# Experts' tokens sorted while attention runs, experts' weights held stationary under 416 streamed rows, and last-layer outputs scattered by token

## The reference, cut to what matters

```python
for t in range(S):                      # B=4, H=8, S=768, D=48; r, k, v: [B, H, S, D]
    cur = einsum('bhd,bhe->bhde', u * kt, vt)
    y[:, :, t] = einsum('bhd,bhde->bhe', rt, state + cur)
    state = w[:, :, None] * state + einsum('bhd,bhe->bhde', kt, vt)
x = y.transpose(0, 2, 1, 3).reshape(3072, 384)        # 3072 tokens
logits = x @ w_gate                                   # 8 experts
e_idx = argmax(logits, axis=1)                        # one expert for each token
gate_w = softmax(logits)[e_idx];  eom = sigmoid(x @ w_output_gate)[e_idx]
for e in range(8):                                    # w1: 384 x 1024, w2: 1024 x 384
    ye = maximum(x[e_idx == e] @ w1[e], 0) @ w2[e]
    x2[e_idx == e] = gate_w * eom * ye
g = x2 @ w_gate2                                      # d_ff = 1536
out = (g * sigmoid(g) * (x2 @ w_val)) @ w_out         # float32
```

## Time and profile before

| | us |
|---|---|
| time, median of 3 runs | 996.05 |
| lowest and highest run | 994.66, 996.93 |
| span of the profiled execution, first to last instruction | 962.4 |

### The profile page before, as it was taken

How to read it: one execution, slowest core, us unless ns; L and a number is a source line. 1 busy time by engine, 2 the same in 40 slices (tenths; PEclk the granted TensorE clock), 3 DMA queues, 4 the chain that set the end, 5 groups by cost and what they waited for, 6 DMA issues and landing times.

```text
span 962.4 us, 19802 instructions
## 1 busy us (share of the span) xinstructions
PE 905.8 (94%) x6919; PEld 856.9 (89%) x6920; DVE 416.5 (43%) x697; ACT 255.9 (27%) x511; POOL 341.3 (35%) x276
## 2 busy tenths in 40 slices
PE   6899998898998999999979999999999999999998
PEld 6777787697897888988878999999999999999998
DVE  7767766536655547264244222222232223222221
ACT  1333332122222222222233222222222222222222
POOL 6799996577444326065346010010100001000000
PEclk9999999999999999999999999999999999999999
DMA  8885565353324132224221010000100001000000
GB/s 198 224 223 129 129 163 186 85 167 113 133 85 155 39 133 82 82 62 150 93 80 29 22 42 9 25 25 0 49 0 25 25 18 31 0 25 0 25 1 25
DMA packets 115583, 74.20 MB, mean 77 GB/s; under 512 B 79248, under 2 KB 109840, under 8 KB 115552
## 3 DMA queue, kind: packets, MB, share of 16 engines
q1 hardware_dynamic: 101312, 48.01, 18.2%
q10 hardware_dynamic: 10720, 14.95, 4.3%
q0 software_dynamic: 3520, 10.82, 4.0%
HBM read 57.44 MB, written 16.32 MB: 77 GB/s over the span
## 4 chain that ended last, share of the span: by engine, by line
PE 67%; POOL 12%; issue 7%; DVE 6%; DMA 3%; POOLq 2%; DVEq 1%; SPq 1%; ACT 1%; ACTq 0%
PE bank L1187 20%; PE bank L1189 20%; PE bank L1188 20%; POOL w_lo L501 3%; POOL w_lo L552 3%; DMA xs<-x_rows,token_of 2%; POOL k_pad L486 2%; POOL r_pad L488 2%; POOL ruk L491 2%; PE bank L1239 1%; PE bank L1083 1%; POOL xs L531 1%; POOLq L549 1%; SPq L401 1%; DVE w_hi L832 1%
## 5 line engine op out<-in xcount | busy, mean ns | idle before, releaser
L1187 PE MATMUL bank<-bT_hi,f_hi 128*128 (+1 forms) x576 | 194.7, 338 | 0.0
L1188 PE MATMUL bank<-bT_lo,f_hi 128*128 (+1 forms) x576 | 192.8, 335 | 0.0
L1189 PE MATMUL bank<-bT_hi,f_lo 128*128 (+1 forms) x576 | 192.6, 334 | 0.0
L890 DVE TENSOR_TENSOR act<-silu,bank 128x384 f32<-128x384 f32 x96 | 53.2, 554 | 252.1 <-PE bank L1189 252.1
L552 POOL TENSOR_TENSOR w_lo<-raw,w_hi x72 | 99.0, 1408 | 111.1 <-DVE w_hi L832 107.0
L571 POOL DMA_INDIRECT xg<-y_slots,slot_of x24 | 25.0, 1040 | 277.4 <-DVE xg_s L874 256.2
L1188 PEld LDWEIGHTS bank<-bT_lo,f_hi 128*128 128x128 f32 x576 | 108.5, 188 | 0.0
L1187 PEld LDWEIGHTS bank<-bT_hi,f_hi 128*128 128x128 f32 x576 | 108.4, 188 | 0.0
L1189 PEld LDWEIGHTS bank<-bT_hi,f_lo 128*128 128x128 f32 x576 | 108.4, 188 | 0.0
L1187 PE MATMUL bank<-f_hi,act_hi 128*128 128x384 f32 x288 | 96.8, 336 | 2.5 <-DVE act_lo L893 2.5
L1189 PE MATMUL bank<-f_hi,act_lo 128*128 128x384 f32 x288 | 96.7, 336 | 0.0
(11 more groups left out here) (169 smaller groups left out, 1464.6 us busy)
## 6 DMA issues: line engine op xcount, KB each, us to landing
raw<-in_moe_w_dram SPq DMA_DIRECT2D x16, 1536.0 KB, 6.7
y_slots<-y_out ACTq DMA_DIRECT2D x28, 192.0 KB, 1.9
k_in<-in_k_dram SPq DMA_DIRECT2D x24, 192.0 KB, 2.7
r_in<-in_r_dram SPq DMA_DIRECT2D x24, 192.0 KB, 3.5
v_in<-in_v_dram SPq DMA_DIRECT2D x24, 192.0 KB, 3.7
x_rows<-x_out ACTq DMA_DIRECT2D x24, 192.0 KB, 1.9
out_dram<-o_out ACTq DMA_DIRECT2D x7, 576.0 KB, 3.0
f_raw<-in_moe_w_gate_dram SPq DMA_DIRECT2D x12, 192.0 KB, 2.6
```

The costliest lines, as they stand in the source:

```text
L890: dve.tensor_tensor(act[:, par, :], silu[:, par, :], bank[2 * par + 1][:, 0:BN], ALU.mult).then_inc(act_made, 1)
L1187: pe.matmul(ps, a_hi, b_hi_, start=first, stop=False)
L1188: pe.matmul(ps, a_hi, b_lo_, start=False, stop=False)
L1189: return pe.matmul(ps, a_lo, b_hi_, start=False, stop=last)
```

## The change

**During attention.** `x_out` holds three chunks, with room for 16 logits behind each row of 384. After each chunk of four steps, VectorE picks the experts of its 512 tokens (`choose`), TensorE counts ranks with three small matmuls (`ranks`), VectorE turns them into row numbers (`place`), and GpSimd scatters the rows with their logits into `x_sorted` in DRAM, a region of 3584 rows for each expert (`store_rows`, one indirect DMA a step, 16 of them between attention steps and 8 behind them). Only one expert's weights are split in attention, in eight chunks of 768 columns, in steps 4 to 11. The attention loops are unrolled.

**Between.** Counts of the tokens give tables of windows of 416 rows. SP writes 416 rows of zeros behind each expert's last row, the first expert's ahead of the first load of rows, the other seven behind it. The one-hot inversion and the gathers are gone.

**Experts.** `window_rounds` loops over windows. A window's rows are loaded as [104, 4] rows by a plain DMA, scaled by their gates at once (`scale_of`, `scale_rows`), transposed by 12 small transposes and split. `up(j, f)` and `down(j, f)` hold 128x128 blocks of the weights stationary and stream the 416 rows, 9 matmuls each; the hidden layer comes out transposed as `down` needs it. All weights of an expert are loaded and split in eight chunks, in the window before. With seed 0 the reference's arithmetic gives the experts 380, 348, 359, 410, 409, 389, 374 and 403 tokens (28 tiles of 128, as the kernel before uses), so each has one window. During the first window GpSimd also issues 24 indirect DMAs that write each sorted row's token number to `token_at` (`place_token`).

**Last layer.** The outputs stay on chip (`y_all`, transposed), so nothing is stored, gathered or transposed. Six blocks of 512 sorted rows; `gate_and_val` streams 512 columns, into the same two PSUM banks each time; `to_out` does 12 matmuls of 384 columns. GpSimd scatters each output tile to `out` by the token numbers (`store_out`).

The diff, cut to its core:

```diff
-    BT = 3
-    BN = BT * P
+    WP, WT = 104, 4
+    W = WP * WT
+    REGION = 3584
+    ROW = DM + 2 * E
+    BN = 512
+    BT = BN // P
...
+            fill(0, first_filled)
+            sp.wait_ge(first_filled, 16)
+            for n in range(XBUF):
+                for b in range(B):
+                    sp.wait_ge(x_stored[n][b], 16 * CH // XBUF)
+            load_rows(0)
+            for e in range(1, E):
+                fill(e, rest_filled)
+            sp.wait_ge(tables_made, 1)
+            end = last_window(sp)
+            sp.wait_ge(rest_filled, 16 * (E - 1))
+            with sp.Fori(1, end + 1, 1) as j:
+                row = sp.value_load(window_row[0:1, bass.ds(j, 1)], min_val=0, max_val=E * REGION - W)
+                sp.wait_ge(xs_made, WT * j)
+                load_rows(row)
+                e = sp.value_load(window_expert[0:1, bass.ds(j, 1)], min_val=0, max_val=E - 1)
+                for f in range(FC1):
+                    sp.wait_ge(w_split, FC1 * j + (f - RAW + 1))
+                    load_chunk(e, f)
...
-                if not at_end(c, 0):
-                    lo_piece(i - B)
+                if SPLIT_AT <= i < SPLIT_AT + FC1:
+                    lo_chunk(0, i - SPLIT_AT)
...
+            for i in range(STEPS):
+                attention_step(i)
+                for n in STORE_AFTER.get(i, ()):
+                    store_rows(n)
...
+            for j, first, last in window_rounds(pool, end):
+                for f in range(FC1):
+                    if f < SPLIT_LAG and not first:
+                        lo_chunk(j, FC1 - SPLIT_LAG + f)
+                    if f >= SPLIT_LAG and not last:
+                        lo_chunk(j + 1, f - SPLIT_LAG)
+                    if first:
+                        for t in range(f * NT // FC1, (f + 1) * NT // FC1):
+                            place_token(t)
+                if first:
+                    pool.wait_ge(tokens_placed, 16 * NT)
...
+            set_routing_up()
+            for i in range(STEPS):
+                attention_step(i)
+                if i >= B and i % B == 1:
+                    choose(i // B - 1)
+                if i >= B and i % B == 2:
+                    place(i // B - 1)
+            choose(CH - 1)
+            place(CH - 1)
...
+            for j, first, last in window_rounds(dve, end):
+                for f in range(FC1):
+                    hidden_lo(j, f)
+                    if f == 1 and not first:
+                        y_copy(j - 1)
+                    if not last:
+                        if f == 0:
+                            scale_of(j + 1)
+                        if f in (1, 2):
+                            scale_rows(j + 1, range((f - 1) * WT // 2, f * WT // 2))
+                        if f in COPY_AT:
+                            x_lo(j + 1, COPY_AT.index(f))
...
+            def up(j, f):
+                pe.wait_ge(w_split, FC1 * j + (f + 1))
+                wait(pe, h_lo_made, FC1 * j + (f - 1))
                 for c in range(KC):
+                    mm = three_passes(bank[f % 2][:, 0:W], w_hi[:, f, at], w_lo[:, f, at],
+                                      window_of(xT_hi, j, c), window_of(xT_lo, j, c), c == 0, c == KC - 1)
...
-                wait(pe, act_made, i - 1)
+                wait(pe, act_made, i)
```

More of the change, by code:

```diff
@@ L867, in _ @@
[L867 to L877 removed]
+            dve.tensor_tensor(place_i[:], place_f[:], slot_f[:], ALU.add).then_inc(places_made, 1)
@@ new lines, in _ @@
+            for c in range(KC):
+                rows_turn(0, c)
+            stay_warm(WARM_FIRST, bank[0])
+            pe.wait_ge(tables_made, 1)
+            end = last_window(pe)
+            for j, first, last in window_rounds(pe, end):
+                for f in range(FC1):
+                    up(j, f)
+                    if f in TURN_AT and not last:
+                        rows_turn(j + 1, TURN_AT.index(f))
+                    if f >= 2:
+                        down(j, f - 2).then_inc(down_mm, 1)
+                    elif not first:
+                        down(j - 1, FC1 - 2 + f).then_inc(down_mm, 1)
```

1192 lines of the change are left out of this document (523 added, 669 removed).

## The result

The changed kernel took 1016.46 us (median of four runs, 1015.08 to 1019.49) beside 995.36 for the kernel before (993.85 to 996.93): ratio 1.0229, 95% interval 1.0200 to 1.0258. It is slower; 921 was forecast, with a range of 901 to 945.

A forecast was written before the change was run, and what follows sets the result against it. TensorE was taken as the main bound, with GpSimd holding attention. The terms 10 + 0 - 57 - 15.9 - 15 + 2.5 = -75.4 took the 962.4 span to 887.0; plus 33.65 outside it, 921 us, range 901 to 945.

The forecast's parts named there:

- Step 1: Attention: GpSimd loses 20 pieces and gains eight wider subtractions and 16 scatters between steps; +10 us.
- Step 2: Routing, from the last `x_out` to the first expert matmul: 24.8 us before and after, change 0, bounds 20 and 29.
- Step 3: Experts: 297.0 to 240 us, -57, from 223.8 of TensorE work and 16.5 of holes.
- (a): First expert window: the second load of rows stands behind seven zero fills, leaving TensorE about 8.5 us idle.
- (c): First expert window: GpSimd's 24 token scatters delay its splits, so the third window's rows come late; 4 us.
- (b): Experts: TensorE's clock drops after the wait before the first window and after (a); twice about 2 us.
- rival B: Late rows hold every expert window, 3.7 us in each of six: 22 us, so 943; chance 0.17.
- Step 4: Hand-over between expert layers: store, gather, scale and transposes go; 18.2 to 2.3 us, -15.9.
- Step 5: Last layer: 72 steps of 6.18 us, fewer matmuls and transposes; 461.2 to 446 us, -15.
- Rival D: Last layer: one pair of PSUM banks makes TensorE wait in each of 72 steps, slower than before; chance 0.04.
- Step 6: The end: four copies, then four scatters 1.30 apart, the last landing 3.3 after its start; 3.8 to 6.3 us, +2.5.
- C: Attention takes its upper bound, VectorE's loop up to about 6 us in steps with `choose`: +14, so 935; chance 0.16.

The follow-up runs named there:

- e1: The changed kernel with GpSimd's weight subtraction in attention one step behind ScalarE's cast; 972.6 us, ratio 1.006 to the kernel before.
- e6: e5_four with each of the 16 scatters in attention one step later; 933.8 us, ratio 0.943 to the kernel before.
- e8: e6 with two buffers for ruk in turn instead of one; 905.1 us, ratio 0.940 to the kernel before.
- e11: e10_spread with two buffers for ruk in turn; 906.4 us, ratio 0.939 to the kernel before.
- e7: e6 with room for four chunks in x_out, so 8 scatters stand between attention steps and 16 behind; 908.0 us, ratio 0.942 to the kernel before.
- e12_best: e6 plus two ruk buffers, room for four chunks in x_out and spread token writes; 898.8 us, ratio 0.930 to the kernel before.
- e2: The changed kernel with the next window's rows issued behind the fifth of eight chunk loads, not the eighth; 976.1 us, ratio 1.008 to the kernel before.
- before_again: The kernel before run once more in the second series, nothing edited; 994.9 us.
- e5_four: The changed kernel with subtraction a step later, next window's rows earlier, token numbers written in the last layer, six zero fills behind window 1's rows; 939.0 us.
- e6_again: e6 run once more in a later series, nothing edited; 913.3 us, ratio 0.944 to the kernel before.
- e10_spread: e6 with the 24 token writes three behind each of the eight late weight slices; 912.4 us, ratio 0.947 to the kernel before.

## Why the prediction was wrong, step by step

**Step 1, attention, +10: the step that failed most, +67.9 measured.** It failed in "It gains eight subtractions of 768 columns, 1.5 times as wide, 2.2 each: +17.6". The subtractions took 1.80 us each, less than the 2.2, and the scatters were near (1.28 to 1.30). What is missing is the wait: I counted the subtraction as busy time of GpSimd and never asked what it waits for, nor who waits for what stands behind it. The diff shows both: `lo_piece(i - B)` became `lo_chunk(0, i - SPLIT_AT)`, the same index as ScalarE's cast, and the cast stood behind `logits_copy`. That is 37 us on the last `x_out` (e1). Of the other 21 over the forecast, some 8 went when the scatters moved a step on (e6; the wait for row numbers that I had as a bound came to 5.0 in e1), 6 to 7 with the second ruk buffer (e8, e11), and scatters taken out of the steps gave 9 (e7); the last `x_out` of one kernel moves by up to 3 us between runs. The floor of 4.4 us a step from the earlier trace rows, 5.7 with a scatter, did not hold as a floor of the step: the twelve steps behind the circle took 6.95 on average, since GpSimd's work is one part of a loop with VectorE and TensorE. e12_best's 164.0 is under the 167.4 forecast, with eight scatters instead of 16 inside.

**Step 2, routing, 0: +4.8.** 29.6 us, 0.6 over the upper bound. The first of the last four scatters started 9.2 us behind the last `x_out` (5.3 in the forecast), the load of rows was issued 8.7 later (7.4) and took 5.8 to land (4.7); scaling took 3.1 (4.6), transposes and two splits 2.9 (2), at half the clock.

**Step 3, experts, -57: -4 measured.** TensorE's 223.8 us of work was some 7 too low: a window without a hole takes 29.0, not 28, and eight about 231, since the last has no rows to transpose. That the best kernels take 240, the number of the forecast, is luck, for the forecast had 16.5 of holes in it; in e12_best 5.4 of the 9 beyond the 231 are waits for scaled rows. Four more terms were wrong. (a) The first gap, 8.5: it was 17.4. The second load of rows was issued, not landed, 26 us behind the first, and took another 8.8 instead of 4.7. The fills themselves were as fast as priced; what I left out are the 4.5 us between their end and the issue. (c) The third window's rows, 4: 12.8. (b) The clock: I gave two gaps 2 us each. "TensorE: Matmul & The Clock Gate" (the Trainium skill, section HAM oscillation) says that a DMA wait in a loop can put the clock down in each iteration; the rows now agree, for a wait that late rows cause: 0.95 over a window with a 3.48 us wait, 1.00 over one without. And the term that I left out of the sum, rival B, came true: 34.4 us a window. Its place was right: the rows were issued 2.0 us before VectorE began the next window (its `hidden_lo(j, 0)`, at 416.39) and landed 4.1 behind that, about as forecast, and the landing that I wanted 6 us longer was not needed. I had read only the first reader, VectorE ahead of `hidden_lo(j, 1)`. The loss sits at the second: ScalarE's casts queue behind exponentials that wait for the same rows, so GpSimd's subtractions and VectorE's scalings meet, and TensorE waits for the scaled rows. e2 took 5.4 us out of each window; I had priced 3.7.

**Step 4, hand-over, -15.9: -14.1. Step 5, last layer, -15: -10.2**, both inside their bounds; step 5 at 6.23 us a step. Rival D did not happen. **Step 6, +2.5: +7.0**. Behind the start of the last scatter, at 1006.63, lie 7.2 us, where I took 3.3. It is not the landing, 2.6 in the median: no DMA moves anything behind 1009, and what the last 4.8 us are is not shown. The sum was also short in itself: three spacings of 1.30 and 3.3 are 7.2, not 6.3.

**The sum's last line, "The 33.65 us between span and median are outside and stay",** failed as well. before_again has them inside the span, as a stall of the kernel before, and the changed kernel does not have that stall. For the executions of the forecast's 996 this is inferred, since none of them has a trace with that time. With it gone, the same steps would have forecast about 890.

**Rivals.** B and C, whose signs came (windows above 30, steps without a weights' piece above 6), had 0.17 and 0.16; I treated them as alternatives, and both came at once, with the cast's wait beside them that was in no rival. The chance of 0.95 for faster rested on the step sizes and not on the order of the instructions, which decided. The best kernel shows that the new structure can be faster (its span of 894.4 is near the forecast 887.0, in part by luck, as above). On the fills, no run settles what "DMA: Bandwidth & Descriptors" (the Trainium skill, on the semaphore increment of 16) says for 104 partitions, since none varies them; the 20.4 us that I worked out from it did not come, for the fills moved at 302 GB/s.

## What to carry to other kernels

When an edit moves an instruction that waits for another engine, write down the distance in steps between producer and consumer before and after; if it falls to zero, follow what stands behind the consumer until you come back to the producer, and price the whole circle instead of the instruction's duration. A DMA that feeds the next iteration is placed by the latest instruction ahead of it in its queue: compare when it lands with when its first reader stands in line, and read the second reader too. Where time and span differ by much more in one kernel than in another, measure the base again before you add the difference to a forecast.

## What the runs showed of the hardware

- The kernel before has two times: 965 to 968 us in three of five comparisons, 992 to 995 in two. In the one trace of the longer kind the difference is time in the first expert tiles in which engines wait for nothing that the profile shows (17.9 and 13.0 us on ScalarE, 13.3 on TensorE). e5_four and e6_four_stores showed the like in the last layer, 15 us. Cause open.
- Four VectorE scalings of 104x384 take 1.41 us where GpSimd rests, and 4.35 to 5.67 beside its subtractions. VectorE's decay of the state had a mean of 793 ns in the kernel before, 868 and 1227 in e6_again and e10_spread, and 1596 in e8_ruk_pair. How busy GpSimd is does not explain this: in attention it was busy for 95% in the kernel before and for 83% in e8_ruk_pair. Which operations meet may; that was not tested. VectorE's operations that read PSUM are not stretched: the hidden residual of the changed kernel takes 559 to 593 ns in all 64, in a stage with 64 of GpSimd's subtractions, and the sum that makes `x_out` 543 to 559 in every trace. "SBUF — State Buffer" (the Trainium skill, section "Who interferes with whom") says that an operation of VectorE in a mode that uses two ports, and one of GpSimd, exclude each other for a whole instruction, and that a VectorE operation with two inputs in SBUF contends with a GpSimd one that reads SBUF; the rows agree in which operations are hit.
- GpSimd's eight subtractions of 768 columns in attention took 1.80 us each, as against 1.49 for 512 columns.
